# The exponential of a causal attention reads its scores from PSUM; VectorE takes only the row maximum

## Chip, cores and metric

The kernel runs on one core of a Trainium2 chip. The metric is device time in microseconds of one execution. Three runs of the kernel before took 1142.82, 1143.03 and 1145.59 us; the median is 1143.03 us.

## The reference, cut to what matters

```python
B, H, S, D = 4, 8, 576, 64
scores = scale * q @ k^T                       # scale = 1/sqrt(64)
cum    = cumsum(max(s, 0))                     # per head, along the sequence
scores = where(causal, -1e9, scores + min(-(cum_i - cum_j), 0))
scores = scores - max(scores, axis=-1)
attn   = exp(scores); attn = attn / (sum(attn) + 1e-9)
x      = attn @ v                              # then (2304 tokens, 512)
x      = rmsnorm(x) * g;  x = (silu(x @ w_gate) * (x @ w_val)) @ w_out
h      = x @ w_in;        out = (h - tanh(h)) @ w_out2
```

Everything is float32. The two feed-forward stages use products split in two parts (fp32r high part and remainder) and take three quarters of the time; the change touches only the attention.

## The kernel before

**Tiling.** Each batch has four pairs of heads, so there are 16 pairs in all. A pair has five query blocks, u = 0 to 4, of 64, 128, 128, 128 and 128 queries, which see 64, 192, 320, 448 and 576 keys. One step n treats one query block of both heads of the pair (hh = 0, 1). The batch loop runs batch 0, a hardware loop over batches 1 and 2, and batch 3. In this text, pairs are numbered 0 to 15.

**The score of a block.** `scores` (L883) lets TensorE write one block into the PSUM tile `SC` (four banks of 512 floats): the high parts (L898), the remainders with the decay rows (L899), and the causal mask by a product with the identity (L903). Blocks 0 and 2 of a pair use bank 0 or 1 (by head), blocks 1 and 3 bank 2 or 3, and block 4, which has 576 keys, needs two banks: 0 and 1 for the first head, 2 and 3 for the second. `score_bank_free` (L100) gives the count after which a bank may be written again. The second head of block 4 needs both banks of block 3, which are those of the step just before it; the first head of the next pair's block 0 needs the bank of the first head of block 4, again the step just before. All other blocks wait for something at least a step and a half older.

**From score to probability.** `minima` (L666) on VectorE copies the score, times -SCALE, from PSUM to the SBUF tile `PR` and gives the row minimum of that as the accumulator output `NM` (L680); the semaphore `mins_done` then counts up. `PR` has four buffers, so the copy also waits until TensorE has transposed the block of four steps ago (`t_done`). `exponential` (L446) on ScalarE works in place on `PR` (L451) and accumulates the row sum `RS`; `exp_done` counts up. TensorE's bank wait (L892) is on `mins_done`.

**The rest of a step.** TensorE's order in step n is: scores(n, 0), transposes(n-2, 0), scores(n, 1), transposes(n-2, 1), `spread` (n-2, L943, the reciprocal sums), `values` (n-3, L931). Transposes (L915) go to two PSUM banks in turn; ScalarE empties even groups (L462), VectorE odd ones (L698). VectorE's order in step n: `output` (n-4, L712), row minimum of head 0, `recip` (n-1: L686 adds an epsilon to the sums, L688 takes the reciprocal), evacuation of n-2, row minimum of head 1, evacuation of n-2, and in some steps `prepare_q` (L664) and `weights` (L720, L722).

**The next pair's operands.** GpSimd's `prepare` (L379) makes the high parts and remainders of the next pair's keys and queries: KA (L388), QO (L390), KD (L393), QA (L394), for head 0 and then head 1, and then KD's decay rows (L402). It starts once all scores of the pair before the current one are done, so after the second head of block 4 (`scores_done`, L385). All orders are written out by hand; there is no planner.

Of the kernel before, what the change touches and what calls it, by code (L numbers as in the profile page):

```python
# [1 line left out]

# [31 lines left out]
F32 = mybir.dt.float32  # L34
F32R = mybir.dt.float32r
BF16 = mybir.dt.bfloat16
ACT = mybir.ActivationFunctionType

P = 128
B, H, S, D = 4, 8, 576, 64  # L40
# [83 lines left out]
def wait(eng, semaphore, count):  # L124

    if not isinstance(count, int) or count > 0:
        eng.wait_ge(semaphore, count)


def build(nc, qT, kT, v, s, w1, w2, g_col, out):  # L130
    ctx = ExitStack()
    with ctx:
        def sem(name):
            return ctx.enter_context(nc.semaphore(name))
# [64 lines left out]
        MP = pb("MP", [P, 2, BANK], F32)  # L199
        MS = MP[:, 1, P:P + CH]  # L200

        def slot(m):

            return WA[:, m] if m < M_ATT else WY[:, m - M_ATT] if m < M1 else WX[:, m - M1 + 2]
# [26 lines left out]
        const_step = sem("const_step"); consts = sem("consts"); cum_step = sem("cum_step")  # L234
        padded = sem("padded"); ones_set = sem("ones_set")
        k_hi = sem("k_hi"); q_hi = sem("q_hi"); q_lo = sem("q_lo")
        scores_done = sem("scores_done"); mins_done = sem("mins_done"); exp_done = sem("exp_done")
        eps_done = sem("eps_done"); recip_done = sem("recip_done")
        spread_mm = sem("spread_mm"); spread_done = sem("spread_done")
        t_done = sem("t_done"); evac_act = sem("evac_act"); evac_dve = sem("evac_dve")  # L240
# [125 lines left out]
        @block.gpsimd  # L366
        def _(pool):
            pool.memset(ident[:], 0.0).then_inc(const_step, 1)
            pool.memset(maskb[:], 0.0).then_inc(const_step, 1)
            pool.wait_ge(const_step, 2)  # L370
            pool.affine_select(out=ident[:], in_=ident[:], compare_op=ALU.not_equal, fill=1.0, base=0,
                               pattern=[[-1, P]], channel_multiplier=1).then_inc(const_step, 1)

            pool.affine_select(out=maskb[:], in_=maskb[:], compare_op=ALU.is_ge, fill=MASKED / SCALE, base=0,
                               pattern=[[-1, P]], channel_multiplier=1).then_inc(consts, 1)
            pool.wait_ge(const_step, 3)
            pool.tensor_copy(identb[:], ident[:]).then_inc(consts, 1)

            def prepare(b, p, hh):  # L379

                j = p % 2
                if hh == 0:
                    pool.wait_ge(qk_in[j], 4 * 16 * (2 * b + p // 2 + 1))

                    wait(pool, scores_done, 2 * (b * STEPS + QB * (p - 1)))  # L385
                    pool.wait_ge(decay_set, b * PAIRS + p)
                    pool.nop(nofuse=True)
                pool.tensor_scalar(KA[:, j, hh], Kraw[:, j, hh], 1.0, 1.0, ALU.mult, ALU.mult  # L388
                                   ).then_inc(k_hi, 1)
                pool.tensor_scalar(QO[0:D, j, hh], Qraw[0:D, j, hh], 1.0, 1.0, ALU.mult, ALU.mult)  # L390
                pool.wait_ge(k_hi, 2 * (b * PAIRS + p) + hh + 1)
                pool.nop(nofuse=True)
                pool.tensor_tensor(KD[0:D, j, hh], Kraw[0:D, j, hh], KA[0:D, j, hh].bitcast(F32), ALU.subtract)  # L393
                pool.tensor_scalar(QA[:, j, hh], Qraw[:, j, hh], 1.0, 1.0, ALU.mult, ALU.mult  # L394
                                   ).then_inc(q_hi, 1)

            def prepare_decay(b, p):

                pool.wait_ge(decay_in, 16 * (b * PAIRS + p + 4))
                pool.wait_ge(q_hi, 2 * (b * PAIRS + p) + 2)  # L400
                pool.nop(nofuse=True)
                pool.tensor_scalar(KD[D:D + 2, p % 2], Draw[D:D + 2], 1.0, 1.0, ALU.mult, ALU.mult  # L402
                                   ).then_inc(decay_set, 1)

            def batch(b, last=False):
                for p in range(PAIRS):
                    if not (last and p == PAIRS - 1):
                        at = (b + (p + 1) // PAIRS, (p + 1) % PAIRS)
                        for hh in range(2):
                            prepare(*at, hh)  # L410
                        prepare_decay(*at)


            pool.wait_ge(qk_in[0], 4 * 16)
            for hh in range(2):
                pool.tensor_scalar(QA[:, 0, hh], Qraw[:, 0, hh], 1.0, 1.0, ALU.mult, ALU.mult).then_inc(q_hi, 1)
            batch(0)
            with pool.Fori(1, B - 1) as b:
                batch(b)
            batch(B - 1, last=True)  # L420


            pool.wait_ge(gcol_in, 16)
            pool.wait_ge(sq_done, KT)
            pool.wait_ge(decay_set, B * PAIRS)
            for t in range(KT):
                x = X[:, t, 0:CH]
                pool.tensor_scalar(x, x, gcol[:, t:t + 1], 1.0, ALU.mult, ALU.mult).then_inc(xg_done, 1)
# [16 lines left out]
        def _(act):  # L445
            def exponential(b, n, hh):  # L446

                _, z, nk, _ = q_block(n % QB)
                pr = PR[0:z, n % 4, hh, PAD:PAD + nk]
                act.wait_ge(mins_done, b * 2 * STEPS + 2 * n + hh + 1)  # L450
                act.activation(pr, pr, ACT.Exp, bias=NM[0:z, n % 4, hh:hh + 1], scale=-1.0,  # L451
                               accum_out=RS[0:z, n % 4, hh:hh + 1]).then_inc(exp_done, 1)

            def evacuate(b, n, hh):
# [54 lines left out]

            act.wait_ge(qk_in[0], 4 * 16)  # L510
            for hh in range(2):
                act.activation(QO[0:D, 0, hh], Qraw[0:D, 0, hh], ACT.Copy)
                act.activation(KA[:, 0, hh], Kraw[:, 0, hh], ACT.Copy).then_inc(k_hi, 1)
            act.wait_ge(decay_in, 16 * 4)
            act.activation(KD[D:D + 2, 0], Draw[D:D + 2], ACT.Copy).then_inc(decay_set, 1)
# [120 lines left out]
        def _(dve):  # L636
# [5 lines left out]
            for j in range(2):  # L642
# [3 lines left out]
            dve.wait_ge(cum_step, 2)  # L646
            dve.tensor_tensor_scan(cum, ones, s_pos, 0.0, ALU.mult, ALU.add).then_inc(cum_step, 1)
            dve.wait_ge(cum_step, 3)
            dve.tensor_scalar(cum_hi, cum, 1.0 / SCALE, None, ALU.mult).then_inc(cum_step, 1)
            dve.wait_ge(cum_step, 4)  # L650
            dve.scalar_tensor_tensor(cum_lo, cum, 1.0 / SCALE, cum_hi.bitcast(F32), ALU.mult, ALU.subtract
                                     ).then_inc(cum_step, 1)
            dve.memset(one_rows, 1.0).then_inc(ones_set, 1)
            dve.wait_ge(ones_set, 1)
            for j in range(2):
# [4 lines left out]
            def prepare_q(b, p, hh):  # L660

                dve.wait_ge(q_hi, 2 * (b * PAIRS + p) + hh + 1)
                q = QA[D:2 * D, p % 2, hh]
                dve.tensor_tensor(q, Qraw[D:2 * D, p % 2, hh], q.bitcast(F32), ALU.subtract).then_inc(q_lo, 1)  # L664

            def minima(b, n, hh):  # L666

                u = n % QB
                _, z, nk, _ = q_block(u)
                dve.wait_ge(scores_done, b * 2 * STEPS + 2 * n + hh + 1)
                wait(dve, t_done, b * NG + groups_of(n - 4, 1)[-1][0] + 1)
                dve.nop(nofuse=True)
                bank = score_bank(u, hh)
                sc = SC[0:z].rearrange("p a f -> p (a f)")[:, bank * BANK:bank * BANK + nk]
                dve.tensor_scalar(PR[0:z, n % 4, hh, PAD:PAD + nk], sc, -SCALE, 3.0e38, ALU.mult, ALU.min,  # L680
                                  accum_out=NM[0:z, n % 4, hh:hh + 1]).then_inc(mins_done, 1)

            def recip(b, n):
                z = q_block(n % QB)[1]
# [55 lines left out]
            def batch(b, first=False, last=False):  # L740
                for n in range(STEPS):
# [1 line left out]
                    if n > V_LAG or not first:  # L743
                        output(b, n - V_LAG - 1)
                    for hh in range(2):
                        minima(b, n, hh)
                        if hh == 0 and (n >= 1 or not first):
                            recip(b, n - 1)
                        if n >= T_LAG or not first:
                            evacuate(b, n - T_LAG, hh)  # L750
                        if last and n == MS_STEP and hh == 0:
                            dve.wait_ge(ms_done, 1)
                            dve.tensor_copy(SQ[:, 0], MS).then_inc(ms_read, 1)
# [125 lines left out]
        def _(pe):  # L879
# [3 lines left out]
            def scores(b, n, hh):  # L883
# [5 lines left out]
                    pe.wait_ge(q_lo, 2 * (b * PAIRS + p + 1))  # L889
                    pe.wait_ge(decay_set, b * PAIRS + p + 1)  # L890

                wait(pe, mins_done, b * 2 * STEPS + score_bank_free(n, hh))  # L892
                pe.nop(nofuse=True)
                bank = score_bank(u, hh)
                sc = SC[0:z].rearrange("p a f -> p (a f)")[:, bank * BANK:]
# [103 lines left out]

            for hh in range(2):  # L1000
                transposes(B, -2, hh)
            pe.wait_ge(mins_done, 2 * B * STEPS)
            pe.wait_ge(w_lo, B * PAIRS)
            gate(0, 0)
            spread(B, -2)
# [113 lines left out]
```

## Time and profile before

| | |
|---|---|
| median of 3 runs | 1143.03 us |
| span of the profiled execution | 1144.2 us |
| time of that execution beyond its span | not given; only the span is known |
| TensorE busy, whole span | 1103.7 us (96%) |
| VectorE busy | 508.3 us (44%) |
| ScalarE busy | 424.8 us (37%) |
| GpSimd busy | 133.0 us (12%) |
| row minimum and copy, L680 | 160 times, mean 486 ns |
| exponential, L451 | 160 times, mean 560 ns |

The attention takes the first 273 us or so of the span; after that TensorE is busy practically without a gap and the lines of the change do not run. Shares over the whole span therefore say little about the change, and what counts is read from the stretch before 273 us. PE's busy time is that of pipelined matmuls, whose ends are modelled; a row's start is the firmer number.

### The profile page before, as it was taken

The numbers are of one execution on the slowest core, as the hardware profiler recorded it, in microseconds if no ns is written. First come the engines' busy times: TensorE is split into PE (matmuls) and PEld (weight loads), VectorE is DVE, ScalarE is ACT, GpSimd is POOL, SyncE is SP. The second block draws the span as 40 slices with busy tenths as digits, with TensorE's granted clock in tenths as the row PEclk, the third lists the DMA queues.
The fourth block names the chain that finished last, engine by engine and source line by source line (L and its number), as shares of the span: only waits on it lengthen the run. The fifth ranks groups of instructions, "written<-read, shape, count | busy, mean of one in ns | idle before, by whom it ended". The sixth has DMA issues, their size and how long they took to land.

```text
span 1144.2 us, 19844 instructions
## 1 busy us (share of the span) xinstructions
PE 1103.7 (96%) x7028; PEld 1010.1 (88%) x7028; DVE 508.3 (44%) x1276; ACT 424.8 (37%) x1031; POOL 133.0 (12%) x162
## 2 busy tenths in 40 slices
PE   4999989989999999999999999999999999999998
PEld 3777767767999999999999999999999999999997
DVE  7789878986443132232232233442323232232322
ACT  3566656665343122222231233442323232232322
POOL 4554445443000000000000000000000000000000
PEclk9999989999999999999999999999999999999999
DMA  6444334411320000000000012220000000000000
GB/s 163 122 124 123 104 84 122 123 33 33 89 65 1 1 1 0 0 0 0 0 1 0 0 55 84 74 84 1 28 1 27 0 27 0 0 27 0 27 0 27
DMA packets 47765, 47.26 MB, mean 41 GB/s; under 512 B 3262, under 2 KB 39102, under 8 KB 47706
## 3 DMA queue, kind: packets, MB, share of 16 engines
q1 hardware_dynamic: 47706, 46.52, 14.9%
q8 instruction: 31, 0.51, 0.2%
q14 instruction: 28, 0.23, 0.1%
HBM read 41.63 MB, written 4.87 MB: 41 GB/s over the span
## 4 chain that ended last, share of the span: by engine, by line
PE 91%; DVE 4%; issue 2%; DMA 1%; SPq 1%; ACT 0%; DVEq 0%; ACTq 0%
PE HP L979 15%; PE HP L977 15%; PE HP L978 15%; PE YP L978 10%; PE YP L977 10%; PE YP L979 10%; PE TP L915 5%; PE OP L931 4%; PE SC L898 3%; PE OP L943 2%; PE SC L899 2%; DVE RE L686 1%; PE SC L903 1%; DVE PR L680 1%; DVE PT L698 1%
## 5 line engine op out<-in xcount | busy, mean ns | idle before, releaser
L977 PE MATMUL HP<-XS,WA 128*128 128x384 f32 x576 | 194.6, 338 | 0.3 <-ACT AC L531 0.3
L979 PE MATMUL HP<-XS,WA 128*128 128x384 f32 x576 | 193.0, 335 | 0.0
L978 PE MATMUL HP<-XS,WA 128*128 128x384 f32 x576 | 192.7, 335 | 0.0
L785 DVE TENSOR_TENSOR AC<-AC,HP 128x384 f32<-128x384 f32 (+2 forms) x78 | 40.3, 523 | 294.4 <-PE HP L979 294.4
L836 DVE TENSOR_TENSOR AC<-HP,AC 128x384 f32<-128x384 f32 (+1 forms) x108 | 54.3, 512 | 215.7 <-ACT AC L593 215.7
L593 ACT ACTIVATE AC<-HP 128x384 f32<-128x384 f32 x96 | 47.2, 492 | 215.2 <-PE HP L979 214.7
L977 PEld LDWEIGHTS HP<-XS,WA 128*128 128x128 f32 x576 | 108.2, 188 | 3.0 <-issue 0.5
L978 PEld LDWEIGHTS HP<-XS,WA 128*128 128x128 f32 x576 | 108.1, 188 | 2.4
L451 ACT ACTIVATE PR<-PR,NM 64x64 f32<-64x64 f32 (+4 forms) x160 | 89.5, 560 | 52.9 <-DVE PR L680 51.1
L979 PEld LDWEIGHTS HP<-XS,WA 128*128 128x128 f32 x576 | 108.1, 188 | 0.0
L915 PE MATMUL TP<-ident,PR 128*128 128x128 f32 (+1 forms) x480 | 88.1, 289 | 16.5 <-DVE PT L698 9.6
L977 PE MATMUL YP<-HS,WX 128*128 128x384 f32 (+2 forms) x312 | 102.1, 327 | 0.7 <-DVE HS L791 0.3
L531 ACT ACTIVATE AC<-HP 128x384 f32<-128x384 f32 x72 | 35.4, 492 | 178.3 <-PE HP L979 178.3
L979 PE MATMUL YP<-HS,WX 128*128 128x384 f32 (+2 forms) x312 | 101.6, 326 | 0.0
L978 PE MATMUL YP<-HS,WX 128*128 128x384 f32 (+2 forms) x312 | 101.5, 325 | 0.0
L979 PE MATMUL HP<-XS,WY 128*128 128x384 f32 x288 | 96.5, 335 | 0.0
L977 PE MATMUL HP<-XS,WY 128*128 128x384 f32 x288 | 96.5, 335 | 0.0
L978 PE MATMUL HP<-XS,WY 128*128 128x384 f32 x288 | 96.4, 335 | 0.0
L898 PE MATMUL SC<-KA,QA 128*64 128x64 f32 (+2 forms) x192 | 72.2, 376 | 14.1 <-DVE QA L664 13.4
L538 ACT ACTIVATE HS<-AC 128x384 fp32r<-128x384 f32 (+2 forms) x78 | 38.8, 500 | 125.1 <-DVE AC L785 125.1
L680 DVE TENSOR_SCALAR_CACHE_REDUCE PR<-SC 64x64 f32<-64x64 f32 (+4 forms) x160 | 77.7, 486 | 12.8 <-PE SC L903 10.6
L850 DVE TENSOR_TENSOR HS<-AC,HS 128x384 fp32r<-128x384 f32 (+1 forms) x108 | 55.5, 514 | 53.7 <-ACT HS L600 51.3
(114 smaller groups left out, 2118.7 us busy)
## 6 DMA issues: line engine op xcount, KB each, us to landing
X<-in_w SPq DMA_DIRECT2D x52, 256.0 KB, 3.2
Kraw<-in_kT SPq DMA_DIRECT2D x32, 288.0 KB, 4.4
Qraw<-in_qT SPq DMA_DIRECT2D x32, 288.0 KB, 5.6
out_rows<-OS SPq DMA_DIRECT2D x18, 256.0 KB, 2.2
Vt<-in_v SPq DMA_DIRECT2D x16, 256.0 KB, 3.0
WRAW<-in_w SPq DMA_DIRECT2D x16, 256.0 KB, 3.1
Vt<-in_v SPq DMA_DIRECT2D x16, 32.0 KB, 1.9
Draw<-cum_scratch SPq DMA_DIRECT2D x15, 9.0 KB
```

Of the source, the lines that this page charges most:

```text
L451: act.activation(pr, pr, ACT.Exp, bias=NM[0:z, n % 4, hh:hh + 1], scale=-1.0, accum_out=RS[0:z, n % 4, hh:hh + 1]).then_inc(exp_done, 1)
L593: act.activation(AC[:, m % 2], HP[:, m % 2, 0:CH], ACT.Tanh).then_inc(tanh_done, 1)
L680: dve.tensor_scalar(PR[0:z, n % 4, hh, PAD:PAD + nk], sc, -SCALE, 3.0e38, ALU.mult, ALU.min, accum_out=NM[0:z, n % 4, hh:hh + 1]).then_inc ...
L785: dve.tensor_tensor(AC[:, m % 2, cols], AC[:, m % 2, cols], HP[:, 1, cols], ALU.mult).then_inc(prod_done if part is None else prod_part, 1)
L836: dve.tensor_tensor(AC[:, m % 2, cols], HP[:, m % 2, cols], AC[:, m % 2, cols], ALU.subtract).then_inc(diff_done if part is None else diff ...
L850: dve.tensor_tensor(HS[:, m % 2, 1, cols], AC[:, m % 2, cols], HS[:, m % 2, 0, cols].bitcast(F32), ALU.subtract).then_inc(glo_done if part ...
L898: pe.matmul(sc[:, keys], QA[:, j, hh, q0:q0 + z], KA[:, j, hh, keys], start=True, stop=False)
L915: last = pe.transpose(TP[:, g % 2, i * P:i * P + z], PR[0:z, n % 4, hh, j * P:(j + 1) * P], ident[0:z, 0:z])
L931: last = pe.matmul(OP[hh * D:(hh + 1) * D, n % 2, 0:z], Vt[:, p % 2, j, hh * D:(hh + 1) * D], PT[:, n % 2, hh, j * P:j * P + z], start=(j ...
L977: pe.matmul(dst, w(0), x(0), start=start, stop=False)
L978: pe.matmul(dst, w(0), x(1), start=False, stop=False)
L979: return pe.matmul(dst, w(1), x(0), start=False, stop=stop)
```

## The change

VectorE no longer copies the score to SBUF. It takes the row maximum with a `tensor_reduce` (negated, into `NM`), and the exponential reads `SC` in PSUM with scale 1.0 and that bias, writing to `PR`. The scale 1/8 moves into the query operands, and the decay sums and the mask lose their factor of 8. The wait for a free `PR` buffer moves from VectorE to ScalarE, with its `nop`. TensorE's bank wait, and one wait after the attention, are now on `exp_done` instead of `mins_done`.

```diff
+        def scores_of(u, hh):
+            _, z, nk, _ = q_block(u)
+            bank = score_bank(u, hh)
+            return SC[0:z].rearrange("p a f -> p (a f)")[:, bank * BANK:bank * BANK + nk]
...
-            pool.affine_select(out=maskb[:], ..., fill=MASKED / SCALE, ...)
+            pool.affine_select(out=maskb[:], ..., fill=MASKED, ...)
...
-                pool.tensor_scalar(QO[0:D, j, hh], Qraw[0:D, j, hh], 1.0, 1.0, ALU.mult, ALU.mult)
+                pool.tensor_scalar(QO[0:D, j, hh], Qraw[0:D, j, hh], SCALE, 1.0, ALU.mult, ALU.mult)
...   (QA the same, in two places; ScalarE's first QO gets scale=SCALE)
             def exponential(b, n, hh):
-                pr = PR[0:z, n % 4, hh, PAD:PAD + nk]
-                act.wait_ge(mins_done, b * 2 * STEPS + 2 * n + hh + 1)
-                act.activation(pr, pr, ACT.Exp, bias=NM[0:z, n % 4, hh:hh + 1], scale=-1.0,
+                act.wait_ge(max_done, b * 2 * STEPS + 2 * n + hh + 1)
+                wait(act, t_done, b * NG + groups_of(n - 4, 1)[-1][0] + 1)
+                act.nop(nofuse=True)
+                act.activation(PR[0:z, n % 4, hh, PAD:PAD + nk], scores_of(n % QB, hh), ACT.Exp,
+                               bias=NM[0:z, n % 4, hh:hh + 1], scale=1.0,
                                accum_out=RS[0:z, n % 4, hh:hh + 1]).then_inc(exp_done, 1)
...
-            dve.tensor_scalar(cum_hi, cum, 1.0 / SCALE, None, ALU.mult).then_inc(cum_step, 1)
+            dve.tensor_copy(cum_hi, cum).then_inc(cum_step, 1)
...   (cum_lo and q_lo: one instruction each, tensor_tensor <-> scalar_tensor_tensor)
-            def minima(b, n, hh):
+            def maxima(b, n, hh):
                 dve.wait_ge(scores_done, b * 2 * STEPS + 2 * n + hh + 1)
-                wait(dve, t_done, b * NG + groups_of(n - 4, 1)[-1][0] + 1)
-                dve.nop(nofuse=True)
-                dve.tensor_scalar(PR[0:z, n % 4, hh, PAD:PAD + nk], sc, -SCALE, 3.0e38, ALU.mult, ALU.min,
-                                  accum_out=NM[0:z, n % 4, hh:hh + 1]).then_inc(mins_done, 1)
+                dve.tensor_reduce(NM[0:z, n % 4, hh:hh + 1], scores_of(u, hh), AX.X, ALU.max, negate=True
+                                  ).then_inc(max_done, 1)
...
             def scores(b, n, hh):        # TensorE
-                wait(pe, mins_done, b * 2 * STEPS + score_bank_free(n, hh))
+                wait(pe, exp_done, b * 2 * STEPS + score_bank_free(n, hh))
...
-            pe.wait_ge(mins_done, 2 * B * STEPS)       # before the first feed-forward product
+            pe.wait_ge(exp_done, 2 * B * STEPS)
```

## Rows read from the trace of the kernel before

**Rows 1.** The page's slices: TensorE's busy tenths, 28.6 us each.
```profile
PE   4999989989999999999999999999999999999998
```

**Rows 2.** One pair: stretch and length, busy us of PE, PEld, DVE, ACT, POOL; clock, DMA.
```profile
115.50:131.10 15.60, 14.51 (x147) 11.37 (x147) 14.07 (x46) 9.74 (x31) 7.77 (x10) 1.00 0.44 115
```

**Rows 3.** Waits from 40 to 275 us: who waited for whom, us, times, longest.
```profile
POOL KA L388 <- PE SC L903: 107.5, 13, 12.7
...
PE TP L915 <- DVE PT L698: 9.6, 12, 0.9
```

**Rows 4.** Timeline, pair 6, blocks 3 and 4: start us, length us, what.
```profile
120.51 0.23 PE L903 MATMUL SC<-maskb,identb 128*128 128x128 bf16 x1
...
120.89 0.62 DVE L680 TENSOR_SCALAR_CACHE_REDUCE PR<-SC 128x448 f32<-128x448 f32 x1 [0.39 <-PE SC L903]
...
121.86 0.62 DVE L680 TENSOR_SCALAR_CACHE_REDUCE PR<-SC 128x448 f32<-128x448 f32 x1
...
122.41 0.08 DVE L680 DVE_READ_ACCUMULATOR PR<-SC 128x1 f32 x1
122.41 0.42 DVE L698 COPY PT<-TP 128x256 f32<-128x256 f32 x1
...
122.52 0.67 ACT L451 ACTIVATE PR<-PR,NM 128x448 f32<-128x448 f32 x1 [0.20 <-DVE PR L680]
...
123.10 0.19 ACT L451 ACTIVATION_READ_ACCUMULATOR PR<-PR,NM 128x1 f32 x1
...
123.15 0.48 PE L898 MATMUL SC<-KA,QA 128*128 128x512 f32 x1
...
123.85 0.24 PE L903 MATMUL SC<-maskb,identb 128*128 128x64 bf16 x2
...
124.33 0.68 POOL L388 TENSOR_SCALAR KA<-Kraw 128x576 fp32r<-128x576 f32 x1 [7.68 <-PE SC L903]
...
125.19 0.24 PE L898 MATMUL SC<-KA,QA 128*64 128x64 f32 x1
...
125.25 0.19 ACT L451 ACTIVATION_READ_ACCUMULATOR PR<-PR,NM 128x1 f32 x1
```

**Rows 5.** Timeline, the same pair's end: GpSimd, VectorE and TensorE in block 1.
```profile
128.88 1.40 POOL L393 TENSOR_TENSOR KD<-Kraw,KA 64x576 fp32r<-64x576 f32 x1
...
129.21 1.10 DVE L686 TENSOR_SCALAR RE<-RS 64x2 f32<-64x2 f32 x1
...
130.51 0.42 DVE L698 COPY PT<-TP 128x256 f32<-128x256 f32 x1
...
131.08 0.41 PE L915 MATMUL TP<-ident,PR 128*128 128x128 f32 x2 [0.82 <-DVE PT L698]
...
131.53 0.42 DVE L698 COPY PT<-TP 128x256 f32<-128x256 f32 x1 [0.32 <-PE TP L915]
```

**Rows 6.** Groups by line and shape: count, busy us, mean ns.
```profile
L698 DVE COPY PT<-TP 128x512 f32<-128x512 f32 x16 | 11.0, 687 | 0.7 <-PE TP L915 0.7
```

**Rows 7.** Timeline, pair 0, second head of block 4.
```profile
27.36 0.77 PE L898 MATMUL SC<-KA,QA 128*128 128x512 f32 x1 [0.74 <-DVE PR L680]
...
27.83 0.19 ACT L451 ACTIVATION_READ_ACCUMULATOR PR<-PR,NM 128x1 f32 x1
```

**Rows 8.** Timeline, the same two instructions in pairs 2, 14 and 15.
```profile
60.89 0.19 ACT L451 ACTIVATION_READ_ACCUMULATOR PR<-PR,NM 128x1 f32 x1
...
61.06 0.48 PE L898 MATMUL SC<-KA,QA 128*128 128x512 f32 x1
...
254.25 0.48 PE L898 MATMUL SC<-KA,QA 128*128 128x512 f32 x1
...
254.60 0.19 ACT L451 ACTIVATION_READ_ACCUMULATOR PR<-PR,NM 128x1 f32 x1
...
270.16 0.48 PE L898 MATMUL SC<-KA,QA 128*128 128x512 f32 x1
...
270.54 0.18 ACT L451 ACTIVATION_READ_ACCUMULATOR PR<-PR,NM 128x1 f32 x1
```

More of the change, by code:

```diff
@@ L37 @@
 ACT = mybir.ActivationFunctionType
+AX = mybir.AxisListType
 P = 128
@@ L236, in build @@
         k_hi = sem("k_hi"); q_hi = sem("q_hi"); q_lo = sem("q_lo")
-        scores_done = sem("scores_done"); mins_done = sem("mins_done"); exp_done = sem("exp_done")
+        scores_done = sem("scores_done"); max_done = sem("max_done"); exp_done = sem("exp_done")
         eps_done = sem("eps_done"); recip_done = sem("recip_done")
@@ L372, in _ @@
                                pattern=[[-1, P]], channel_multiplier=1).then_inc(const_step, 1)
-            pool.affine_select(out=maskb[:], in_=maskb[:], compare_op=ALU.is_ge, fill=MASKED / SCALE, base=0,
+            pool.affine_select(out=maskb[:], in_=maskb[:], compare_op=ALU.is_ge, fill=MASKED, base=0,
                                pattern=[[-1, P]], channel_multiplier=1).then_inc(consts, 1)
@@ L393, in prepare @@
                 pool.tensor_tensor(KD[0:D, j, hh], Kraw[0:D, j, hh], KA[0:D, j, hh].bitcast(F32), ALU.subtract)
-                pool.tensor_scalar(QA[:, j, hh], Qraw[:, j, hh], 1.0, 1.0, ALU.mult, ALU.mult
+                pool.tensor_scalar(QA[:, j, hh], Qraw[:, j, hh], SCALE, 1.0, ALU.mult, ALU.mult
                                    ).then_inc(q_hi, 1)
@@ L415, in _ @@
             for hh in range(2):
-                pool.tensor_scalar(QA[:, 0, hh], Qraw[:, 0, hh], 1.0, 1.0, ALU.mult, ALU.mult).then_inc(q_hi, 1)
+                pool.tensor_scalar(QA[:, 0, hh], Qraw[:, 0, hh], SCALE, 1.0, ALU.mult, ALU.mult).then_inc(q_hi, 1)
             batch(0)
@@ L511, in _ @@
             for hh in range(2):
-                act.activation(QO[0:D, 0, hh], Qraw[0:D, 0, hh], ACT.Copy)
+                act.activation(QO[0:D, 0, hh], Qraw[0:D, 0, hh], ACT.Copy, scale=SCALE)
                 act.activation(KA[:, 0, hh], Kraw[:, 0, hh], ACT.Copy).then_inc(k_hi, 1)
@@ L648, in _ @@
             dve.wait_ge(cum_step, 3)
-            dve.tensor_scalar(cum_hi, cum, 1.0 / SCALE, None, ALU.mult).then_inc(cum_step, 1)
+            dve.tensor_copy(cum_hi, cum).then_inc(cum_step, 1)
             dve.wait_ge(cum_step, 4)
-            dve.scalar_tensor_tensor(cum_lo, cum, 1.0 / SCALE, cum_hi.bitcast(F32), ALU.mult, ALU.subtract
-                                     ).then_inc(cum_step, 1)
+            dve.tensor_tensor(cum_lo, cum, cum_hi.bitcast(F32), ALU.subtract).then_inc(cum_step, 1)
             dve.memset(one_rows, 1.0).then_inc(ones_set, 1)
@@ L663, in prepare_q @@
                 q = QA[D:2 * D, p % 2, hh]
-                dve.tensor_tensor(q, Qraw[D:2 * D, p % 2, hh], q.bitcast(F32), ALU.subtract).then_inc(q_lo, 1)
-            def minima(b, n, hh):
+                dve.scalar_tensor_tensor(q, Qraw[D:2 * D, p % 2, hh], SCALE, q.bitcast(F32), ALU.mult, ALU.subtract
+                                         ).then_inc(q_lo, 1)
+            def maxima(b, n, hh):
                 u = n % QB
@@ L675, in minima @@
                 dve.wait_ge(scores_done, b * 2 * STEPS + 2 * n + hh + 1)
-                wait(dve, t_done, b * NG + groups_of(n - 4, 1)[-1][0] + 1)
-                dve.nop(nofuse=True)
-                bank = score_bank(u, hh)
-                sc = SC[0:z].rearrange("p a f -> p (a f)")[:, bank * BANK:bank * BANK + nk]
-                dve.tensor_scalar(PR[0:z, n % 4, hh, PAD:PAD + nk], sc, -SCALE, 3.0e38, ALU.mult, ALU.min,
-                                  accum_out=NM[0:z, n % 4, hh:hh + 1]).then_inc(mins_done, 1)
+                dve.tensor_reduce(NM[0:z, n % 4, hh:hh + 1], scores_of(u, hh), AX.X, ALU.max, negate=True
+                                  ).then_inc(max_done, 1)
             def recip(b, n):
@@ L745, in batch @@
                     for hh in range(2):
-                        minima(b, n, hh)
+                        maxima(b, n, hh)
                         if hh == 0 and (n >= 1 or not first):
```

## Prediction, made before the changed kernel was timed

> **What bounds the kernel now.** I read the page's slices first. TensorE is 90% busy or more nearly everywhere; only in the first ten slices, the attention, is there room [rows 1], so the change can act only there. The busy times of one regular pair come next: of 15.6 us, TensorE works 14.5, VectorE 14.1, ScalarE 9.7 and GpSimd 7.8 [rows 2]. Two engines are nearly full, so I do not trust the sums and look at the waits. TensorE's one repeated long wait is for VectorE's evacuation L698, 12 times, 9.6 us in all, 0.8 us each; the largest wait of all is GpSimd's KA for the last score of a pair, 13 times [rows 3].
>
> The timeline ties these together. The second head of block 4 (I call it S) starts at 123.15 and its mask product ends at 123.85 + 0.24 = 124.09; GpSimd's KA starts at 124.33 [rows 4]. GpSimd then runs its chain through to the second KD, 128.88 to 130.28. VectorE's tiny L686, two elements wide, starts at 129.21 and ends at 130.31, that is 0.03 after KD ends: it was held while GpSimd's KD ran. Then come the reciprocal, the evacuation from 130.51 to 130.93, and TensorE's transpose at 131.08, after 0.82 idle [rows 5]. From there TensorE runs to the next S. So in a regular pair the loop is: S, 1.2 us to KA, 5.95 us of GpSimd, 0.8 of VectorE and its handover, 7.65 of TensorE, together 15.6. A delay of S is a delay of the whole pair, although TensorE idles 0.8 us later on; a delay of the blocks after S is swallowed by that idle time.
>
> **The change, part by part.**
>
> *The bank wait.* This is the term that counts. S may start today once VectorE has read block 3. After the change it also has to wait for block 3's second exponential. In pair 6 that exponential starts at 122.52 and its accumulator read, which releases `exp_done`, ends at 123.10 + 0.19 = 123.29, which is 0.14 later than S starts today [rows 4]. A late release also costs the handover, which a wait that is already satisfied does not: the evacuation ending at 130.93 let TensorE go at 131.08, so 0.15 us [rows 5]. S slips by 0.14 + 0.15 = 0.29 in pair 6.
> I read the same two times in all 16 pairs. Pairs 4 to 11 are like pair 6: late by 0.12, 0.12, 0.14, 0.11, 0.12, 0.12, 0.12 and 0.13, in sum 0.98, plus 8 x 0.15 = 2.18 us. Pairs 1 to 3 are late by 0.05, 0.02 and 0.03 (pair 2: 61.08 against 61.06 [rows 8]), plus 3 x 0.15 = 0.55. Pair 12: 0.04 + 0.15 = 0.19. Pair 13's exponential is 0.58 early: nothing. Pair 0: 28.02 against 27.36 [rows 7], 0.66 + 0.15 = 0.81, and TensorE itself sets the pace there. Pair 14: 254.79 against 254.25, pair 15: 270.72 against 270.16 [rows 8], so 0.54 and 0.56, plus 0.15 each: 0.69 and 0.71. Behind pair 15 the first feed-forward product now waits for the last exponential too, which moves by the same slip, so it is no second term. Sum: 0.81 + 0.55 + 2.18 + 0.19 + 0.69 + 0.71 = 5.1 us.
>
> *The second tight wait.* Block 0 of the next pair waits for the first exponential of block 4: that ends at 125.25 + 0.19 = 125.44, block 0 starts at 125.19 [rows 4]. With the handover it slips by 0.40, only 0.11 more than S already brings. What is queued behind it are transposes, spread and values, and then the transpose with 0.82 idle ahead of it. I count 0; without that cover it would be 0.11 x 12 = 1.3 us. The other score blocks have a microsecond or more.
>
> *The maximum in place of the copy.* The accumulator read of 0.08 disappears 160 times, but it starts at the same 122.41 as the next instruction, the evacuation [rows 4]: it covers no time of its own, and I take 0 for it. A `tensor_reduce` does not occur in the trace. Nearest is a copy from PSUM, 687 ns for 512 columns [rows 6]; the present form takes 624 for 448 (0.62 in [rows 4]), 63 ns less for 64 columns less. Both take one element a cycle, so I expect the same for the maximum. Bounds: it could save the 0.08, or cost about as much more. Block 3's two maxima both lie in front of the exponential that holds S, so this is 0.16 either way per pair, over the 12 regular pairs: the sum becomes 2.8 (it cannot go below no slip in pairs 1 to 3 and 12) or 7.0 us.
> The Trainium skill, "VectorE: DVE Perf Modes", section "Rules for kernel authors", speaks against the change: expect 1x of `tensor_reduce`, the slowest VectorE operation. By that rule a form with a faster mode is given up. The rows show one element a cycle already, so by the rule and by the rows the term is 0 here.
>
> *The nop and the second wait* leave VectorE and go to ScalarE. With them VectorE's reduction started 0.15 after the mask ended (120.74 to 120.89 [rows 4]); without them an evacuation started 0.04 after its transposes (131.49 to 131.53 [rows 5]). The first maximum starts 0.11 earlier, the exponential as much later: 0 for S. The added condition itself, four steps old, never waits.
>
> *The exponential from PSUM.* Same columns, same count. I take 0; one or two hundredths either way. The Trainium skill, "VectorE: DVE Perf Modes", section "The TRN2 errata", gives ScalarE a fixed 224 cycles from SBUF and 172 from PSUM. By that, an estimate, each exponential ends 0.04 earlier and the sum would be 4.6; no row before shows an exponential from PSUM.
>
> *The scale factors* change constants of instructions that exist already; cum_hi and cum_lo run once. 0 us.
>
> So the forecast is +5.1 us. Made against the profiled span, 1144.2 becomes 1149.3; that span stands 1.2 above the median of the runs, and I carry the difference over: 1143.0 + 5.1 = **1148.1 us**.
>
> **The rivals.**
>
> *The idle time swallows it.* TensorE stands 0.82 us before the transpose of block 1 [rows 5], more than the 0.40 it slips. If VectorE's own queue, and not GpSimd, sets the evacuation, the regular pairs cost nothing and pairs 0, 14 and 15 remain: 2.2 us, 1145.2. For it: VectorE is 90% busy. Against it: L686 ends 0.03 after KD, and 1.10 us for two elements is no queue.
>
> *Faster, by the order of L686 and KD.* L686 comes 0.33 us after the second KD has started and then loses 1.10. If it came first, it would be over in 0.17, and TensorE's 9.6 us of waits [rows 3] would go: less the 5.1, the sum is -4.5, 1138.6 us. It decides once GpSimd's chain slips 0.33 more than VectorE's way to L686, or VectorE arrives that much earlier. For it: S's slip moves KD by 0.29, and maxima of block 0 and 1 may start earlier. Against it: L686 stands behind a maximum that needs block 1's scores, and these slip by 0.40, more than KD.
>
> *VectorE's load is what counts*, and the saved accumulator reads come back, 0.08 x 10 a pair, up to 0.8 us x 12: about -4 with the slip. The coinciding starts speak against it; I give it a share of the faster case.
>
> **How the numbers follow.** About 0.3%, 3.4 us, is what a measurement of this kernel can tell from none. Forecast: 0.62, with its own range from 2.8 to 7.0 us, that is 1145.8 to 1150.0; some four fifths of it lies above 3.4. Idle time swallows it: 0.20, all within 0.3%. Faster: 0.10. The last 0.08 is a larger slip, when the maximum is dear and the second wait is felt as well: 7.0 + 1.3, up to 1151.5. Slower: 0.62 x 0.8 + 0.08 = 0.58; same: 0.20 + 0.12 = 0.32; faster: 0.10. The range leaves out the faster case and the far end: 1142.0 to 1150.5.
>
> **What would show it.** Right: a wait of TensorE's L898 for the exponential, 0.1 to 0.3 us before S and again before block 0, in nearly every pair; pairs of 15.8 to 15.9 us instead of 15.6; L686 still about 1 us long in block 1; the maximum at 0.6 us for 448 columns. Wrong: KA starting no later relative to the transpose before it; L686 in front of KD and short; the wait of 9.6 us gone; or exponentials so much earlier that S does not wait.

## The result, and the profile after

The changed kernel takes 1149.59 us (median of six runs, 1148.67 to 1149.77); six runs of the kernel before beside it have a median of 1145.61 (1142.82 to 1146.26). The ratio is 1.0045, 95% interval 1.0033 to 1.0057: slower by about 4.0 us. The forecast was 1148.1, slower by 5.1. The time was inside the range, and above the forecast although the loss was below it: the three runs that I started from lay low (see "The base" below).

The page of the kernel after: the busy times (us, share of the span, count) and TensorE's slices.

```profile
PE 1103.0 (96%) x7028; PEld 1009.9 (88%) x7028; DVE 504.3 (44%) x1116; ACT 420.7 (37%) x1031; POOL 133.0 (12%) x162
...
PE   4999979999999999999999999999999999999998
```

TensorE, VectorE and ScalarE are a little less busy than before, and the kernel is slower: these totals say nothing of the change. One digit of the slices fell, the sixth: 7 where it was 8 [rows 1]. That slice is 143.5 to 172.2 us. The batch loop returns just before it, at 141.3 us on VectorE, and the standstill behind the return fills its start.

The waits of the kernel after, 40 to 276 us (who waited for whom: us, times, longest):

```profile
PE TP L890 <- DVE PT L673: 9.2, 11, 1.2
...
PE OP L918 <- DVE X L687: 6.2, 1, 6.2
...
PE SC L873 <- ACT PR L434: 2.4, 5, 0.8
```

The waits for VectorE's evacuation, 9.6 us before [rows 3], are still there with 9.2, and the new bank wait is in the list with 2.4 us. The wait of 6.2 us for VectorE's `output` is a single one; before, its longest was 3.3 (shown below).

The timeline of pair 6, to be laid beside [rows 4, 5] (start us, length us):

```profile
121.37 0.62 DVE L655 TENSOR_REDUCE NM<-SC 128x1 f32<-128x448 f32 x1 [0.27 <-PE SC L878]
...
122.20 0.62 DVE L655 TENSOR_REDUCE NM<-SC 128x1 f32<-128x448 f32 x1
...
122.94 0.64 ACT L434 ACTIVATE PR<-SC,NM 128x448 f32<-128x448 f32 x1
...
123.48 0.19 ACT L434 ACTIVATION_READ_ACCUMULATOR PR<-SC,NM 128x1 f32 x1
...
123.81 0.47 PE L873 MATMUL SC<-KA,QA 128*128 128x512 f32 x1
...
129.54 1.40 POOL L375 TENSOR_TENSOR KD<-Kraw,KA 64x576 fp32r<-64x576 f32 x1
129.64 1.32 DVE L661 TENSOR_SCALAR RE<-RS 64x2 f32<-64x2 f32 x1
...
131.53 0.42 DVE L673 COPY PT<-TP 128x256 f32<-128x256 f32 x1 [0.38 <-issue]
...
132.10 0.41 PE L890 MATMUL TP<-ident,PR 128*128 128x128 f32 x2 [1.25 <-DVE PT L673]
```

S starts at 123.81, 0.14 after the accumulator read ends (123.48 + 0.19 = 123.67). So it does wait for the exponential, with the handover that I priced. It holds in every pair but pair 13. The tiny operation in block 1 is held as before, 1.32 us. The TensorE idle time behind it is 1.25 here; in the regular pairs it is 0.9, and pair 6 has 0.38 of `issue` on VectorE on top (the word is explained below).

From S of pair to S of pair, in us, read off TensorE's rows in the timelines (the number is the pair that the stretch ends in):

| kernel | 1 | 2, 3 | 4 to 6 | 7 | 8 | 9, 10 | 11 | 12 | 13 | 14 | 15 | S of pair 15 at |
|---|---|---|---|---|---|---|---|---|---|---|---|---|
| before | 18.29 | 15.40 | 15.57 | 15.59 | 20.54 | 15.57 | 15.57 | 15.38 | 16.53 | 16.35 | 15.91 | 270.16 |
| after | 17.97 | 15.40 | 15.61 | 16.00 | 23.03 | 15.62 | 15.97 | 15.41 | 16.40 | 16.84 | 15.76 | 274.47 |

Of the 4.31 us, pair 0 brings 0.85, the six pairs 4, 5, 6, 9, 10 and 12 together only 0.25, pairs 7 and 11 0.4 each, and **pair 8 alone 2.49**. The ends nearly cancel: pair 1 -0.32, pair 13 -0.13, pair 14 +0.49, pair 15 -0.15. Pair 8 is the first after the return of the batch loop. There stands, before and then after:

```profile
145.69 0.29 DVE L712 TENSOR_TENSOR X<-OP,RB 128x128 f32 x1 [3.60 <-issue]
...
146.13 0.69 PE L943 MATMUL OP<-ident,RR 128*64 128x128 f32 x4 [3.31 <-DVE X L712]
```

```profile
145.26 0.28 ACT L452 ACTIVATE RB<-OP 128x128 f32<-128x128 f32 x1 [2.49 <-issue]
...
149.54 0.29 DVE L687 TENSOR_TENSOR X<-OP,RB 128x128 f32 x1 [7.26 <-issue]
...
149.98 0.70 PE L918 MATMUL OP<-ident,RR 128*64 128x128 f32 x4 [6.16 <-DVE X L687]
```

`issue` means that the engine waited for nothing that the profile shows. VectorE stands 3.60 us before and 7.26 after, and TensorE, which waits for its `output`, 3.31 and 6.16. The windows (length, PE busy, matmuls, granted clock, DMA share, GB/s), before and then after, show what follows: the granted clock is 0.50, the lower level of 1.2 GHz, behind the pause, and it stays there longer in the kernel after, where the pause was longer.

```profile
144.00:148.00 4.00, 1.87 (x16) 0.71 0.48 125
148.00:152.00 4.00, 4.00 (x24) 0.50 0.01 2
152.00:156.00 4.00, 4.00 (x50) 0.93 0.01 2
156.00:160.00 4.00, 4.00 (x36) 1.00 0.43 137
```

```profile
144.00:148.00 4.00, 0.00 (x0) 0.68 0.72 178
148.00:152.00 4.00, 2.02 (x17) 0.50 0.03 6
152.00:156.00 4.00, 4.00 (x26) 0.54 0.00 0
156.00:160.00 4.00, 4.00 (x50) 1.00 0.00 0
```

The trace also has the records of VectorE's sequencer, the part that takes its instructions in (count, ns, first and last start). In the kernel before it ends the loop's branch at 141.2 and shows its next record at 145.4. In the kernel after it ends the branch at 141.4, has one record at 145.1 and the next at 149.3. First before, then after:

```profile
L770 DVEq FUSED_REGOPS  x1: 63/63/63, 145.4 to 145.4; - x1
```

```profile
L745 DVEq FUSED_REGOPS  x1: 63/63/63, 145.1 to 145.1; - x1
...
L686 DVEq EVENT_SEMAPHORE  x1: 21/21/21, 149.3 to 149.3; - x1
```

So behind the pause of 7.26 us are two standstills of the sequencer in a row, of 3.7 and 4.2 us (in the first 0.9 us VectorE still works off what it has), each about as long as the single one of 4.15 before.

### The profile page after: what moved, and what is told of

The parts are those of the page before. It is cut to its first block, busy times and chain, and to the rows that moved or that the text cites. A ratio compares the mean times of both kernels' runs of the same rounds, so it can differ in the third digit from the quotient of the medians.

```text
span 1147.9 us, 19718 instructions
## 1 busy us (share of the span) xinstructions
PE 1103.0 (96%) x7028; PEld 1009.9 (88%) x7028; DVE 504.3 (44%) x1116; ACT 420.7 (37%) x1031; POOL 133.0 (12%) x162
## 4 chain that ended last, share of the span: by engine, by line
PE 92%; DVE 4%; issue 2%; DMA 1%; SPq 1%; ACT 0%; ACTq 0%; DVEq 0%
PE HP L952 15%; PE HP L954 15%; PE HP L953 15%; PE YP L953 10%; PE YP L954 10%; PE YP L952 10%; PE TP L890 4%; PE OP L906 4%; PE SC L873 3%; PE OP L918 2%; PE SC L874 2%; DVE RE L661 1%; PE SC L878 1%; DVE NM L655 1%; DVE PT L673 1%
## 5 line engine op out<-in xcount | busy, mean ns | idle before, releaser
L434 ACT ACTIVATE PR<-SC,NM 64x64 f32<-64x64 f32 (+4 forms) x160 | 83.8, 524 | 45.7 <-DVE NM L655 41.8
L655 DVE TENSOR_REDUCE NM<-SC 64x1 f32<-64x64 f32 (+4 forms) x160 | 77.3, 483 | 9.8 <-PE SC L878 8.7
```

The source lines that it names most:

```text
L434: act.activation(PR[0:z, n % 4, hh, PAD:PAD + nk], scores_of(n % QB, hh), ACT.Exp, bias=NM[0:z, n % 4, hh:hh + 1], scale=1.0, accum_out=RS ...
L655: dve.tensor_reduce(NM[0:z, n % 4, hh:hh + 1], scores_of(u, hh), AX.X, ALU.max, negate=True).then_inc(max_done, 1)
```

## The experiments

All times are medians of the same kind, ratios are to runs of the kernel before on the same chip. Theory A is the forecast (S waits for the exponential); the rivals are theory B, that something else in the step moved, and theory C, that the pause at the loop's return, and not the regular pairs, makes the difference.

**1. The bank wait alone.** The kernel before, with only TensorE's two waits changed.

```diff
-                wait(pe, mins_done, b * 2 * STEPS + score_bank_free(n, hh))
+                wait(pe, exp_done, b * 2 * STEPS + score_bank_free(n, hh))
...
-            pe.wait_ge(mins_done, 2 * B * STEPS)
+            pe.wait_ge(exp_done, 2 * B * STEPS)
```

> Only TensorE's two bank waits move to the exponential; VectorE still copies the score. Slip theory: nothing brings the exponential forward here, so the second head of block 4 starts 0.15 us after the exponential of block 3 ends and the full forecast appears: regular pairs of 15.8 us instead of 15.6, about +5 us in all. Rival (the loss of the full change sits at the return of the batch loop, where VectorE waits for its instructions): VectorE's code is as before, so that gap stays near its 3.6 us and the total is +2 us or less.

Measured: 1149.75 us, ratio 1.0036 (1.0024 to 1.0048), so 4.2 us, and not 2 or less. Its regular pairs take 15.83 instead of 15.57 us, pairs 2 and 3 15.56 instead of 15.40, pair 8 19.95. Without pair 8 the slips add up to 4.90 us; 1.43 of that is pair 14. Pair 5 and pair 6 in its timeline:

```profile
109.52 0.47 PE L898 MATMUL SC<-KA,QA 128*128 128x512 f32 x1
...
124.44 0.67 ACT L451 ACTIVATE PR<-PR,NM 128x448 f32<-128x448 f32 x1 [0.20 <-DVE PR L680]
...
125.01 0.19 ACT L451 ACTIVATION_READ_ACCUMULATOR PR<-PR,NM 128x1 f32 x1
...
125.34 0.47 PE L898 MATMUL SC<-KA,QA 128*128 128x512 f32 x1
```

125.01 + 0.19 = 125.20, and S at 125.34: the handover is 0.14. 125.34 - 109.52 = 15.82. The slip of 0.26 a pair is the one that theory A counted as 0.27. **So in the regular pairs the bank wait costs what was forecast, and the rest of the change must give most of it back there**, where the kernel after has +0.04 to +0.06. That the whole sum agrees as well, 4.90 for 5.1, is partly luck. The granted clock fell in this trace in pair 14, and not in those of before and after:

```profile
249.30:252.60 3.30, 3.30 (x25) 0.50 0.01 5
```

In the five kernels of this document whose traces show such a fall there, pair 14 takes 17.48 to 17.78 us; in the other eight 15.91 to 17.02.

**2. The same with more in VectorE's program.** After, with the old wait and the `nop`, but behind the maximum.

```diff
+                wait(dve, t_done, b * NG + groups_of(n - 4, 1)[-1][0] + 1)
+                dve.nop(nofuse=True)
```

> The changed kernel with the removed wait and nop put back on VectorE, but behind the maximum, so that VectorE's code has the old length and the maximum still wakes up fast. Code theory: the gap of VectorE at the batch loop's return goes from 7.3 us back to about 3.6, and 2.5 to 3.5 us of the loss come back. Slip theory: the gap is chance or has another cause, the total stays at +4 to +5 us and the pairs stay at 15.6.

Measured: 1148.57 us, ratio 1.0034 (1.0021 to 1.0047). Regular pairs 15.61 (as after), pairs 7 and 11 15.60 and 15.63 (the 0.4 is gone), pair 8 21.27 instead of 23.03. Neither theory came out: VectorE's pause went to 5.34 us and not to 3.6, and 1 us of the loss came back, not 2.5 or more. Behind the maximum the `nop` costs nothing, in front of it (experiment 4) it does.

**3. ScalarE's new wait and `nop` left out.**

```diff
-                wait(act, t_done, b * NG + groups_of(n - 4, 1)[-1][0] + 1)
-                act.nop(nofuse=True)
```

> The changed kernel without the wait for the free buffer and its nop on ScalarE (ScalarE's order covers that wait already). Handover theory: each exponential that waits for a maximum starts about 0.05 to 0.1 us earlier, the bank is free that much earlier, and regular pairs shorten by as much: -0.5 to -1 us against the changed kernel. Rival: the nop costs nothing and the pairs stay at 15.6.

Measured: 1152.91 us, ratio 1.0067 (1.0055 to 1.0079), the slowest of all. Yet its regular pairs are 15.57, those of before: from the maximum's end to the exponential's end it takes 0.08 less, and S doesn't wait. That is 0.04 a pair, and the smaller total that I expected from it did not come. The loss lies in pair 7 (18.90), pair 8 (22.17) and pair 11 (17.42). In the stretch to pair 7 TensorE has a wait of 1.32 us in block 1, and behind it a granted clock of 0.50:

```profile
132.38 0.41 PE L888 MATMUL TP<-ident,PR 128*128 128x128 f32 x2 [1.32 <-DVE PT L671]
...
132.00:136.00 4.00, 3.62 (x27) 0.67 0.01 4
136.00:140.00 4.00, 4.00 (x29) 0.50 0.00 0
140.00:144.00 4.00, 4.00 (x35) 0.98 0.42 139
```

The stretch is 3.3 us longer than a regular one (18.90 - 15.57), mostly by the lower clock. The kernel after waited 1.25 us at this place, with the same 0.38 of `issue` on VectorE, and kept its clock. But the length of one wait does not decide it: in pair 14 TensorE stood 1.60 us in the kernel before and kept its clock, and 1.61 in that of experiment 1 and lost it. What tips it is not shown.

**4. VectorE's wait and `nop` left out, before.**

```diff
-                wait(dve, t_done, b * NG + groups_of(n - 4, 1)[-1][0] + 1)
-                dve.nop(nofuse=True)
```

> The kernel before, only without the wait for the free buffer and its nop on VectorE (VectorE's order covers it). Handover theory: the row minimum starts 0.1 us after the scores instead of 0.15, and the exponential of block 3 ends 0.1 to 0.2 earlier relative to the block-4 scores; nothing waits for it here, so regular pairs stay at 15.4 to 15.6. Code theory: VectorE's code is as short as in the changed kernel, so the gap at the loop's return rises from 3.6 towards 7.3 us and the kernel gets 2 to 3 us slower.

Measured: 1143.75 us, ratio 0.9985 (0.9975 to 0.9994). Pair 5 of it:

```profile
105.34 0.62 DVE L678 TENSOR_SCALAR_CACHE_REDUCE PR<-SC 128x448 f32<-128x448 f32 x1 [0.27 <-PE SC L901]
...
106.20 0.62 DVE L678 TENSOR_SCALAR_CACHE_REDUCE PR<-SC 128x448 f32<-128x448 f32 x1
...
107.44 0.19 ACT L451 ACTIVATION_READ_ACCUMULATOR PR<-PR,NM 128x1 f32 x1
...
107.73 0.48 PE L896 MATMUL SC<-KA,QA 128*128 128x512 f32 x1
```

Two reductions 0.86 apart (0.97 before: 120.89 and 121.86 [rows 4]), the first of them 0.27 behind the mask's release instead of 0.39. From the transpose of block 1 to the end of block 3's exponential it takes 5.26 + 0.86 + 1.43 = 7.55 us; before, 5.36 + 0.96 + 1.44 = 7.76. The read ends at 107.63 and S starts 0.10 later without having waited: TensorE's own order takes 7.64. The regular pairs stay at 15.6, and the gain is in pair 8, 19.17. The code theory failed: the pause is 4.20 us and not near 7.3, and the kernel is faster and not slower. (It keeps the accumulator reads that the kernel after lacks, so its program is a little longer than that one's.)

**5. The scale of the tiny operation.** Four kernels without L686: the reciprocal reads `RS` itself. The kernels leave out the epsilon of 1e-9 on sums of at least 1.

```diff
-                dve.tensor_scalar(RE[0:z, n % 4], RS[0:z, n % 4], SUM_EPS, None, ALU.add).then_inc(eps_done, 1)
-                dve.wait_ge(eps_done, b * STEPS + n + 1)
-                dve.reciprocal(RR[0:z, n % 4], RE[0:z, n % 4]).then_inc(recip_done, 1)
+                dve.reciprocal(RR[0:z, n % 4], RS[0:z, n % 4]).then_inc(recip_done, 1)
```

From the kernel before:

> The kernel before without L686: the reciprocal reads the row sums themselves (a row sum is at least 1, and 1 + 1e-9 is 1 in float32, so the numbers stay). Lock theory: L686 is what GpSimd's KD holds up in block 1, the reciprocal is not held, TensorE's 0.8 us of idle time per regular pair goes, pairs take 14.8 instead of 15.6 us and the whole is 8 to 10 us faster. Rival (VectorE's load sets the evacuation): one short instruction less per step, 0.2 us, pairs of 15.4 at best and 2 to 3 us in all.

The same with the bank wait of experiment 1:

> Like the one before, with TensorE's bank waits on the exponential as the only other edit. Cover theory: with TensorE's idle time gone, the second tight wait (block 0 for the first exponential of block 4) is felt too. Against the kernel without L686: pairs longer by 0.3 to 0.4 us, +5 to +6 in all. Rival: only the wait ahead of block 4's second head counts; without L686 between the two maxima its exponential ends 0.2 earlier, and pairs are longer by 0.1 or less.

From the kernel after:

> The changed kernel without L686. Lock theory: TensorE's idle time goes here too, pairs of 14.8 to 15.1 us instead of 15.6, 6 to 10 us faster than the changed kernel, and faster than the kernel before. Cover theory: still 0.1 to 0.3 us per pair slower than the kernel before without L686. Rival (VectorE's load): pairs of 15.4 at best.

From the kernel before without VectorE's wait and `nop` (experiment 4):

> The kernel before without VectorE's nop and buffer wait and without L686: the candidate that beats both. If both savings add, pairs of 14.3 to 14.45 us and 0 to 2 us below the 1130 of the kernel without L686 alone; if something else than VectorE's handovers sets the pair of 14.45, no gain, within 1 us.

| kernel | us | ratio | regular pair | pair 8 |
|---|---|---|---|---|
| before, no L686 | 1130.16 | 0.9870 (0.9852 to 0.9888) | 14.45 | 20.31 |
| and bank wait | 1132.65 | 0.9883 (0.9867 to 0.9900) | 14.46 | 20.14 |
| after, no L686 | 1131.47 | 0.9871 (0.9853 to 0.9888) | 14.44 | 19.89 |
| before, no L686, no `nop` | **1124.00** | 0.9813 (0.9798 to 0.9828) | 14.45 | 14.44 |

The end of a pair in the first of them:

```profile
119.78 1.41 POOL L393 TENSOR_TENSOR KD<-Kraw,KA 64x576 fp32r<-64x576 f32 x1
119.86 0.15 DVE L686 RECIPROCAL RR<-RS 64x2 f32<-64x2 f32 x1
120.02 0.42 DVE L696 COPY PT<-TP 128x256 f32<-128x256 f32 x1
120.43 0.74 PE L913 MATMUL TP<-ident,PR 128*128 128x128 f32 x5 [0.18 <-ACT PT L462]
```

The reciprocal of two elements takes 0.15 us although KD runs, and TensorE's 0.8 of idle time is gone. Which operation it is decides, not its being small or on VectorE. A pair becomes 1.12 us shorter, more than the 0.8 expected. With the loop through L686 broken, the bank wait costs 0.01 a regular pair, and after and before are equal, 14.44 and 14.45. Outside the regular pairs it is still felt: pairs 2 and 3 take 14.54 instead of 14.35 with it, pair 12 14.66 instead of 14.34. This bears out the loop that the prediction started from (S, GpSimd, L686, evacuation, transpose, S), and refutes what the expectations added, that without the idle time the second tight wait would be felt. The last kernel is faster than both kernels of this case, by 1.9% and 2.2%; most of the rest of its gain is pair 8, which is as short as a regular pair, with no fall of the clock in the attention:

```profile
145.01 0.48 PE L894 MATMUL SC<-KA,QA 128*128 128x512 f32 x1
...
130.00:140.00 10.00, 9.82 (x101) 1.00 0.63 169
140.00:150.00 10.00, 10.00 (x107) 1.00 0.52 129
```

**6. The pause at the loop's return.** It is shown in the table below for every kernel. First theory: it grows where VectorE's program is shorter. Tested with two waits and two `nop`s behind each maximum, with the same without L686, and with 64 times a satisfied wait and a `nop` at the very start of VectorE's program, ahead of the loop, which leaves the loop's length alone.

```diff
+                wait(dve, t_done, b * NG + groups_of(n - 4, 1)[-1][0] + 1)
+                dve.nop(nofuse=True)
+                dve.wait_ge(scores_done, b * 2 * STEPS + 2 * n + hh + 1)
+                dve.nop(nofuse=True)
```

> The changed kernel with two waits and two nops behind each maximum on VectorE, so that VectorE's program is about as long as before, the accumulator reads counted. Code-length theory: VectorE's gap at the loop's return is 3.6 to 3.9 us as in the kernel before and the one with only the bank wait, and the loss is about 2 us, from the first pairs. Rival (where blocks of code begin, or the transfers beside them, decide, and length alone says nothing): the gap stays above 4.5 us or moves to another place.

> The changed kernel without L686, with the two nops behind each maximum on VectorE. Padding theory: it helps only where it shortens the gap at the loop's return, which is 3.7 us here without it, so no gain: 1130 to 1132 us. Rival (a longer program is as such better): 2 to 4 us faster than without the nops.

```diff
+            for _ in range(64):
+                dve.wait_ge(padded, 1)
+                dve.nop(nofuse=True)
```

> The changed kernel with 64 nops at VectorE's start, outside the loop, so the loop's length stays and only its place in the program moves. Place theory: VectorE's gap at the loop's return changes by more than 1 us from 7.3, and the extra 0.4 us hold in front of block 1's evacuation in pair 6 moves or goes. Length theory: both stay.

Measured: 1146.45 us, 1.0004 (0.9995 to 1.0014); 1133.63 us, 0.9897 (0.9880 to 0.9913); 1149.45 us, 1.0039 (1.0021 to 1.0057). The length theory asked for a pause of 3.6 to 3.9 us in the first and got 4.23; the second is not faster for its padding; in the third the pause moved and the 0.4 of pair 7 went, as the theory of place asked. The idle time is VectorE's, marked `issue`, ahead of its first `output` after the return.

| kernel | VectorE idle | pair 8 |
|---|---|---|
| before | 3.60 | 20.54 |
| bank wait alone | 3.86 | 19.95 |
| before, no `nop` | 4.20 | 19.17 |
| after | 7.26 | 23.03 |
| after, no ScalarE `nop` | 7.03 | 22.17 |
| after, padded | 5.34 | 21.27 |
| after, padded twice | 4.23 | 19.94 |
| after, padded ahead of the loop | none | 18.72 |
| before, no L686 | 4.39 | 20.31 |
| bank wait, no L686 | 4.32 | 20.14 |
| after, no L686 | 3.68 | 19.89 |
| after, no L686, padded twice | 4.59 | 20.38 |
| before, no L686, no `nop` | none | 14.44 |

The row of the kernel padded ahead of the loop:

```profile
150.28 0.28 ACT L452 ACTIVATE RB<-OP 128x128 f32<-128x128 f32 x1 [3.69 <-issue]
```

With the same loop body, padding ahead of the loop takes VectorE's pause away. ScalarE's is then the longest, 3.69 (2.49 in the kernel after), and pair 8 is 18.72 instead of 23.03. **So the loop's length alone does not set the pause, and the padding ahead of it moves the pause.** The length alone doesn't: after without L686 has a shorter program on VectorE than after, and pauses 3.68 and not more than 7.26. The padding moves the loop's place in the program, but it also starts all of VectorE's work later, and no run separates the two. It is no gain in all: it starts pair 0's S at 31.94 instead of 28.21, which eats what pair 8 gives. Padded twice behind the maximum, the change costs nothing that can be measured: pairs 7 and 11 are regular, 15.62, and pair 8 is 19.94.

The DMA queues have two that carry instructions, q8 and q14. Their packets (count, MB, share): before, 141 to 145.3 us; then after, 141 to 145 and 145 to 149.3; then the kernel without a pause, 128 to 150, which has none of q14:

```profile
q14 instruction: 1, 0.01, 0.8%
```

```profile
q14 instruction: 2, 0.02, 2.4%
...
q14 instruction: 2, 0.02, 1.0%
```

```profile
q8 instruction: 1, 0.02, 0.5%
```

Each standstill has its packets. Before, one starts at 143.08, and VectorE goes on at 145.38. After, two start at 143.00 and 143.24, and VectorE goes on at 145.10 and ScalarE at 145.17; two more start at 147.44 and 147.51, and the two engines go on at 149.33 and 149.27. So an engine goes on about 2 us after a packet's start (not every packet has a standstill beside it), and VectorE pauses about twice as long after as before because it stops twice. After without ScalarE's `nop` shows the same pattern: 7.03 us, two stops, packets at 147.08 and 150.47. The number of packets alone does not give the length: after without L686 has 8 from 128 to 150 us and pauses 3.68. The Trainium skill, "Runtime: NRT & Kernel Launch", section "Instruction fetch mechanics", says that a taken branch whose target isn't in the window of code at hand forces a fetch before execution goes on. The packets agree with it, and so does the pause that moves with the padding ahead of the loop. No run here shows which code is fetched, nor why VectorE stops once in one kernel, twice in another and not at all in a third.

## Why the prediction was right and wrong

**Right: the loop and the bank wait.** The bank wait alone slips 0.26 a regular pair (0.27 forecast) and 0.17 in pairs 2 and 3 (0.18), with a handover of 0.14. S waits in the kernel after as well, but its regular pairs are 15.6 and not the 15.8 to 15.9 that I named as the sign. The hold of the two-element operation by GpSimd is what closes the loop: without it a pair is 14.45. The rival that VectorE's queue sets the evacuation falls with that. The rival that L686 comes first came true in block 3 alone, where it takes 0.16 instead of 0.57. In block 1 it starts at 129.64, 0.10 after KD; it would have had to come first. The count behind that step was right by 0.1 us only.

The Trainium skill, "SBUF — State Buffer", section "Who interferes with whom", gives the lock: `tensor_scalar` can take the port pair that VectorE and GpSimd share, whoever issues first holds it for its whole instruction, the other is fully blocked. The rows agree with that: 1.10 and 1.32 us for two elements behind KD. In its place the reciprocal takes 0.15.

**Right: the maximum.** The same shape, 448 columns, before and then after, for its 30 blocks from 40 to 275 us (count, busy us, mean ns, idle time before and what ended it):

```profile
L451 ACT ACTIVATE PR<-PR,NM 128x448 f32<-128x448 f32 x30 | 20.1, 669 | 6.0 <-DVE PR L680 5.5
L680 DVE TENSOR_SCALAR_CACHE_REDUCE PR<-SC 128x448 f32<-128x448 f32 x30 | 18.7, 624 | 5.5 <-PE SC L903 5.0
```

```profile
L434 ACT ACTIVATE PR<-SC,NM 128x448 f32<-128x448 f32 x30 | 19.0, 634 | 4.6 <-DVE NM L655 3.0
L655 DVE TENSOR_REDUCE NM<-SC 128x1 f32<-128x448 f32 x30 | 18.6, 620 | 3.8 <-PE SC L878 3.7
```

620 ns against 624: the term was 0. The lower end that I gave for it does not follow from its own working: 5.1 less 12 x 0.16 is 3.2, and not 2.8. The measured 4.0 lies above both.

**Mis-sized: the exponential from PSUM.** I took 0, one or two hundredths. It is 35 ns shorter here (669 to 634), 41 at 64 columns (343 to 302). The estimate from the figures of the Trainium skill, "VectorE: DVE Perf Modes", section "The TRN2 errata", was 0.04 each, and the rows agree with it.

**Failed: the `nop` and the second wait, "0 for S".** This is the step of the sum that was wrong in the regular pairs. I argued that the maximum's 0.11 earlier is the exponential's 0.11 later. But two maxima and only one exponential lie on the way to S, and VectorE loses more to its `nop` than ScalarE to its own. Experiment 4 gives 0.21 back (7.76 to 7.55 us from the transpose of block 1 to the end of block 3's exponential), and experiment 3 puts ScalarE's at 0.08. With the shorter exponential, 0.04, and some hundredths in the rest, the exponential ends 0.2 earlier: 5.26 + 0.83 + 1.46 = 7.55 instead of 7.76. With 0.15 of handover that is 7.70 to S, where TensorE's own order took 7.64. So a regular pair has +0.04 to +0.06 instead of +0.27, and pairs 2 and 3 have 0. Over pairs 2 to 7 and 9 to 12 (7 and 11 from the padded kernel of experiment 2) it took back 2.0 of the bank wait's 2.3 us. The same figures correct my rule that a release which comes in time costs nothing: this one comes 0.09 before TensorE's own order would start S, and S still slips 0.06. The price is lateness plus handover also where the release is early by less than the handover.

**Missing: the return of the loop.** Pair 8's pause of 3.60 stands in the trace of before, and I read the pairs around it without asking what ends it. The sum had no term for it, so it stood at nothing without a reason. It grew to 7.26, VectorE stopping twice instead of once, and with the lower clock after it pair 8 costs 2.49, more than all the other pairs of the loop together. The 0.4 in pairs 7 and 11 is `issue` on VectorE too, at the same place of the loop body in both of its passes, and absent in all padded kernels; whether it has the same cause is not shown.

**Pair by pair for the rest.** Pair 0: 0.85 (0.81 forecast). Pair 1: -0.32 (0.20 forecast). It follows the clock: the trace's record of the upper level begins 9.1 us behind pair 0's S before and 8.0 after, and over all thirteen kernels, from 3.2 us (pair 1 15.76) to 10.2 (18.72), pair 1 grows with this time, to within 0.2. Pair 14: 0.49 (0.69), pair 15: -0.15 (0.71 forecast); why they came out lower was not tested. In the regular pairs the second tight wait was rightly 0, for another reason than the idle time: it costs nothing without that either (experiment 5).

**The base.** I found the profiled span 1.2 above the median and carried the difference. In the later runs the device time lies 1.8 us above the span (2.0 in one kernel), so the profiled 1144.2 was an execution of about 1146.0, and the three runs' median of 1143.0 was 2.6 below that of six. The forecast of 1148.1 was closer to the 1149.6 than its parts deserve: +5.1 for a measured +4.0, of which +2.5 came from a place that was not in the sum: the number is luck, the bank wait is not.

## What to carry to other kernels

Where a consumer takes over the release of a buffer, price the wait at lateness plus one handover (0.15 us here), also where it is early by less than that, and then count every instruction ahead of it on its way, the `nop`s and second waits too, each as often as it lies on that way and not once. Find the loop that sets the pace first, and look in it for a tiny operation that is held by another engine: one `tensor_scalar` on two elements per step cost 15 us here, far more than the whole change. Look at every stretch marked `issue`, above all behind a hardware loop's return, and at where the granted clock changes: edits shifted both here, and only a comparison pair by pair keeps them apart from what the edit does. The bank wait alone and the whole change have nearly the same total (1149.75 and 1149.59 us) by different pairs.

## What the runs showed of the hardware

- At the return of a hardware loop an engine can stand 0 to 7.3 us; 64 waits and `nop`s ahead of the same loop body took 7.26 us from VectorE, and gave ScalarE 3.69 instead of 2.49. A pause of 7.26 was two stops, of 3.7 and 4.2 us, and each ended about 2 us after a packet of the instruction queue q14 had started.
- TensorE's granted clock fell to 0.50 behind a wait of 1.32 us in one kernel and held at one of 1.25 in another; it also held behind one of 1.60 in the kernel before, and fell behind one of 1.61 with the bank wait alone. The stretch with the fall behind 1.32 us was 3.3 us longer.
- An exponential from PSUM is 35 to 41 ns shorter than one in place in SBUF (669 to 634 and 343 to 302 ns). A `tensor_reduce` and a `tensor_scalar` with accumulator output take the same from PSUM (620 and 624 ns for 448 columns), and the `tensor_reduce` has no read of the accumulator, which is 75 to 83 ns.
- A VectorE `tensor_scalar` of two elements is held while GpSimd works (1.10 us before, 1.32 after, behind KD), a reciprocal of the same two is not (0.15).

**What stays open:** what is fetched at the loop's return, and why VectorE stops there once, twice or not at all; whether the pauses in pairs 7 and 11 have the same cause; and what sets the moments at which the granted clock rises ahead of pair 1 and falls in pair 14. Each kernel has one trace, so how much its pauses vary from run to run isn't known.
